# A delta-rule attention with two feed-forward networks: sums of squares in two reduced-precision parts, and the last output tile finished, copied and stored in parts

## The reference

```python
def _moe2_ref(x, w_gate, w_val, w_out, rms_g):        # x: 3072 x 384
    rms = np.sqrt(np.mean(x * x, axis=-1, keepdims=True) + 1e-06)
    xn = x / rms * rms_g
    g = xn @ w_gate                                   # 384 x 1536
    silu = g * (1.0 / (1.0 + np.exp(-g)))
    val = xn @ w_val                                  # 384 x 1536
    return (silu * val @ w_out).astype(np.float32)    # 1536 x 384
```

## Time and profile before

| | us |
|---|---|
| median of 3 executions | 1063.65 |
| the three executions | 1062.71, 1063.65, 1069.65 |
| the profiled execution, device time | 1068.47 |
| its span, first to last instruction | 1066.6 |
| TensorE busy in it | 1039.2 (97%) |
| VectorE busy | 535.0 (50%) |
| ACT busy | 468.8 (44%) |

### The profile page before, as it was taken

The page is one execution under the profiler, slowest core; times in us unless marked ns, Lnnn a source line. Parts: engine busy times, 40 slices in busy tenths (PEclk is TensorE's granted clock), DMA queues, the critical chain, the costliest instruction groups (busy, mean ns, idle before and its releaser), DMA issues.

```text
span 1066.6 us, 25024 instructions
## 1 busy us (share of the span) xinstructions
PE 1039.2 (97%) x11132; PEld 856.3 (80%) x11132; DVE 535.0 (50%) x1001; ACT 468.8 (44%) x843; POOL 9.6 (1%) x20
## 2 busy tenths in 40 slices
PE   8889899999999999999999999999999999999996
PEld 4469888777777877777778888888888888888885
DVE  6648667747846837753356444324333333333322
ACT  5744654574473474464466542232232232232211
POOL 1000000000000000000000000000000000000000
PEclk9889999999999999999999999999999999999999
DMA  9405102301500410030021230200200100100101
GB/s 258 133 2 130 22 3 62 89 3 37 115 2 3 120 31 3 32 119 3 28 93 49 70 119 1 60 1 1 60 1 13 48 1 1 30 1 1 30 1 30
DMA packets 19034, 48.09 MB, mean 45 GB/s; under 512 B 2448, under 2 KB 9232, under 8 KB 17872
## 3 DMA queue, kind: packets, MB, share of 16 engines
q1 hardware_dynamic: 18800, 46.11, 16.0%
q10 hardware_dynamic: 128, 0.39, 0.1%
HBM read 37.06 MB, written 9.44 MB: 44 GB/s over the span
## 4 chain that ended last, share of the span: by engine, by line
PE 92%; ACT 3%; DMA 2%; issue 1%; DVE 1%; SPq 0%; DVEq 0%; ACTq 0%
PE bank L713 21%; PE hps L1257 19%; PE acc L1272 19%; PE acc L732 10%; PE hps L713 7%; PE hps L732 4%; DMA stage<-w_in 1%; PE acc L1294 1%; PE bank L1216 1%; PE bank L1151 1%; PE bank L1180 1%; PE bank L1202 1%; PE bank L1195 1%; PE bank L1229 1%; PE bank L1141 1%
## 5 line engine op out<-in xcount | busy, mean ns | idle before, releaser
L630 ACT ACTIVATE g<-bank 128x512 f32<-128x512 f32 x72 | 43.2, 600 | 257.2 <-PE bank L713 142.6
L1257 PE MATMUL hps<-xh,w1h 128*128 128x512 f32 (+1 forms) x336 | 129.5, 385 | 2.7 <-DVE g L1089 2.1
L1272 PE MATMUL acc<-g1h,w2h 128*128 128x512 f32 (+1 forms) x336 | 127.0, 378 | 0.4 <-ACT x2s L941 0.3
L1257 PE MATMUL hps<-xl,w1h 128*128 128x512 f32 (+1 forms) x336 | 122.4, 364 | 0.0
L1257 PE MATMUL hps<-xh,w1l 128*128 128x512 f32 (+1 forms) x336 | 122.2, 364 | 0.0
L1272 PE MATMUL acc<-g1l,w2h 128*128 128x512 f32 (+1 forms) x336 | 122.0, 363 | 0.0
L1272 PE MATMUL acc<-g1h,w2l 128*128 128x512 f32 (+1 forms) x336 | 121.8, 363 | 0.0
L933 ACT ACTIVATE g1h<-g 128x512 fp32r<-128x512 f32 (+1 forms) x112 | 64.0, 571 | 120.6 <-DVE g L1089 105.5
L1097 DVE TENSOR_TENSOR g1l<-g,g1h 128x512 fp32r<-128x512 f32 (+1 forms) x112 | 68.6, 612 | 91.5 <-ACT g1h L933 91.1
L1089 DVE SCALAR_TENSOR_TENSOR g<-hps,g 128x512 f32<-128x512 f32 (+1 forms) x112 | 68.2, 609 | 61.6 <-ACT g L927 61.4
L924 ACT ACTIVATE g<-hps,half_c 128x512 f32<-128x512 f32 (+1 forms) x112 | 69.8, 623 | 54.0 <-PE hps L1257 53.2
(11 more groups left out here) (183 smaller groups left out, 2039.9 us busy)
## 6 DMA issues: line engine op xcount, KB each, us to landing
kqT<-kq SPq DMA_DIRECT2D x22, 384.0 KB, 6.6
v_in<-v SPq DMA_DIRECT2D x6, 768.0 KB, 4.3
k_in<-k SPq DMA_DIRECT2D x6, 768.0 KB, 5.6
x2d<-x2s SPq DMA_DIRECT2D x18, 256.0 KB, 5.2
x2t<-x2d SPq DMA_DIRECT2D x6, 768.0 KB, 5.5
y<-y_t SPq DMA_DIRECT2D x48, 96.0 KB, 2.2
stage<-w_in SPq DMA_DIRECT2D x4, 768.0 KB, 9.9
stage<-w_out SPq DMA_DIRECT2D x4, 768.0 KB, 7.6
```

The source lines that it names most:

```text
L630: act.activation(silu[:, f % 2, :], gps[f % 2][:, :], ACT.Silu).then_inc(e_silu, 1)
L1257: last = pe.matmul(hps[f % 2][:, 0:WIDTH[n]], wt[:, kk, P * f:P * f + P], xx[:, kk, COLS[n]], start=(kk == 0 and e == 0), stop=(kk == KD - ...
L1272: last = pe.matmul(acc[j][:, 0:WIDTH[n]], wt[:, f, P * j:P * j + P], gg[:, f % 2, 0:WIDTH[n]], start=(f == 0 and e == 0), stop=(f == NF1 - ...
```

## The change

The sum of squares goes through the high and low parts too. After `fold`, ACT copies the folded squares into an fp32r tile `sumh` (`sumhi`), VectorE subtracts it into `suml` (`sumlo`), and `sums` is two fp32r matmuls with fp32r ones in place of one fp32 matmul. The tile of ones is written by ACT at the start and no longer by POOL. In the last step, y of the last block runs the eight matmuls with `prh` first, behind a wait for `prh` alone, then the four with `prl`, each of which completes a group and signals it. VectorE copies groups 0 and 2, ACT groups 1 and 3; SP issues the four stores of the half m = 0, ACT those of m = 1.

```diff
@@ -260,8 +260,8 @@
     n = TILES - 1
     high, low = [("w2h", n, p) for p in range(15)], [("w2l", n, p) for p in range(15)]
     beside = {("h", n, 0): [("square", 0, 0)], ("h", n, 1): [("square", 0, 1)],
-              ("gl", n, 1): [("square", 0, 2), ("fold", 0, 0)],
-              ("h", n, 2): high[0:1], ("gl", n, 2): high[1:2] + low[0:2], ("h", n, 3): high[2:3], ("gl", n, 3): high[3:4] + low[2:4],
+              ("gl", n, 1): [("square", 0, 2), ("fold", 0, 0), ("sumhi", 0, 0)],
+              ("h", n, 2): high[0:1], ("gl", n, 2): high[1:2] + [("sumlo", 0, 0)] + low[0:2], ("h", n, 3): high[2:3], ("gl", n, 3): high[3:4] + low[2:4],
               ("o", n, 2): [("sums", 0, 0)], ("gl", n, 4): [("root", 0, 0)], ("h", n, 5): high[4:5],
               ("gl", n, 5): [("invert", 0, 0)], ("gl", n, 6): [("invert", 0, 1)], ("h", n, 7): high[5:6],
               ("gl", n, 7): [("scale", 0, 0)], ("h", n, 8): high[6:7], ("gl", n, 8): [("hi", 0, 0)] + low[4:6],
@@ -279,7 +279,7 @@
 def second_network():
-    norms = {2: ["square"], 3: ["fold"], 4: ["sums", "root"], 6: ["invert"], 7: ["invert"], 8: ["scale"], 9: ["hi"], 10: ["lo"]}
+    norms = {2: ["square"], 3: ["fold", "sumhi", "sumlo"], 4: ["sums", "root"], 6: ["invert"], 7: ["invert"], 8: ["scale"], 9: ["hi"], 10: ["lo"]}
     parts = {0: (15, 17), 1: (17, 19), 2: (19, 20), 3: (20, 21), 4: (21, 22), 5: (22, 24), 6: (24, 26), 7: (26, 27)}
     out = []
     for n in range(NSTEP):
@@ -322,7 +322,7 @@
         w2h = sb("w2h", [P, NF1, DM], F32R)
         w2l = sb("w2l", [P, NF1, DM], F32R)
         half_c = sb("half_c", [P, 1])
-        ones = sb("ones", [P, P])
+        ones = sb("ones", [P, P], F32R)
         eps_c = sb("eps_c", [P, 1])
         gain = sb("gain", [P, KD])
         x2s = sb("x2s", [P, KD, T])
@@ -375,9 +375,10 @@
         y_t = sb("y_t", [P, NT4, DM])
         xn0h = sb("xn0h", [P, KD, T], F32R)
         xn0l = sb("xn0l", [P, KD, T], F32R)
+        sumh, suml = sb("x2_sum_hi", [P, T], F32R), sb("x2_sum_lo", [P, T], F32R)
         e_gain, e_x, e_w = sem("gain_loaded"), sem_pair("x2_loaded"), sem_pair("w2_loaded")
         e_wh, e_wl = sem("w2_hi_ready"), sem("w2_lo_ready")
-        e_half, e_fold = sem("x2_half_folded"), sem("x2_folded")
+        e_half, e_fold, e_fh, e_fl = sem("x2_half_folded"), sem("x2_folded"), sem("x2_sum_high"), sem("x2_sum_low")
         e_sq, e_ss, e_rms, e_rinv, e_xs = (sem("x2_squared"), sem("x2_summed"), sem("rms_ready"), sem("rms_inverted"),
                                            sem("x2_normed"))
         w2_raw = {"gate": w_gate.rearrange("(k p) f -> p k f", p=P), "value": w_val.rearrange("(k p) f -> p k f", p=P),
@@ -463,7 +464,7 @@
             by_vector = {("GK", 0, 0): (s_gk2, 1), ("GK", 0, 1): (s_gk2, 2), ("U", 0, 0): (s_upd2, 1), ("PU", 0, 0): (s_y2, 1)}
-            N_CONST = 1 + MEM + 5
+            N_CONST = 1 + MEM + 4
             N_ZERO = 3
             N_NRM = 5
             N_INV = 2 + 2 * INV
@@ -553,6 +554,7 @@
             e_gv, e_silu, e_pr, e_prh, e_prl = (sem("gate_val_done"), sem("silu_ready"), sem("product_ready"),
                                                 sem("product_hi"), sem("product_lo"))
             e_y, e_yc, e_out = sem("y_done"), sem("y_copied"), sem("y_stored")
+            e_ylast, e_ya = sem("y_last_done"), sem("y_last_copied")
             y_rows = y_out.rearrange("(bp m s) n -> bp m s n", bp=BP, m=MEM)
             N_OUT = NT4 * MEM * 16
@@ -566,18 +568,32 @@
                     sp.wait_ge(e_xl, n - 1)
                 sp.dma_start(x2t[n % 2][:, :, :], x2d[n, :, :, :]).then_inc(e_x[n % 2], 16)
+
+            def y_store(eng, n, j, m):
+                hf, bp = j // BP, j % BP
+                eng.dma_start(y_rows[bp ^ m, m, n * STEP + hf * C:n * STEP + hf * C + C, :], y_t[C * m:C * m + C, j, :])\
+                    .then_inc(e_out, 16)
+
+            def last_out_ready(eng, j):
+
+                if j % 2:
+                    eng.wait_ge(e_ya, j // 2 + 1)
+                else:
+                    eng.wait_ge(e_yc, (NSTEP - 1) * NT4 + j // 2 + 1)
             def second_sync(sp):
                 load_x2(sp, 2)
                 load_x2(sp, 3)
                 for n in range(NSTEP):
                     for j in range(NT4):
-                        hf, bp = j // BP, j % BP
+                        if n == NSTEP - 1:
+                            last_out_ready(sp, j)
+                            y_store(sp, n, j, 0)
+                            continue
                         sp.wait_ge(e_yc, n * NT4 + j + 1)
                         for m in range(MEM):
-                            sp.dma_start(y_rows[bp ^ m, m, n * STEP + hf * C:n * STEP + hf * C + C, :], y_t[C * m:C * m + C, j, :])\
-                                .then_inc(e_out, 16)
+                            y_store(sp, n, j, m)
                     if n + 4 < NSTEP:
                         load_x2(sp, n + 4)
@@ -611,6 +627,9 @@
                         act.wait_ge(e_ss, n)
                     act.activation(x2sq[:, :, :], x2t[n % 2][:, :, :], ACT.Square).then_inc(e_sq, 1)
+                elif kind == "sumhi":
+                    act.wait_ge(e_fold, n + 1)
+                    act.activation(sumh[:, :], x2sq[:, 0, :], ACT.Copy).then_inc(e_fh, 1)
                 elif kind == "root":
                     act.wait_ge(e_ss, n + 1)
                     act.activation(rms[:, :], sums_of(n)[:, :], ACT.Sqrt, bias=eps_c[:, 0:1], scale=1.0 / DM).then_inc(e_rms, 1)
@@ -622,6 +641,14 @@
                 elif kind == "hi":
                     act.wait_ge(e_xs, n + 1)
                     act.activation(xnh[n % 2][:, :, :], x2t[n % 2][:, :, :], ACT.Copy).then_inc(e_xh, 1)
+                elif kind == "out" and n == NSTEP - 1:
+                    act.wait_ge(e_out, n * N_OUT)
+                    for j in range(1, NT4, 2):
+                        act.wait_ge(e_ylast, j + 1)
+                        act.activation(y_t[:, j, :], yps[j][:, 0:DM], ACT.Copy).then_inc(e_ya, 1)
+                    for j in range(NT4):
+                        last_out_ready(act, j)
+                        y_store(act, n, j, 1)
                 elif kind == "silu":
                     act.wait_ge(e_gv, n * NF2 + f + 1)
                     if n == 0 and f < 2:
@@ -654,6 +681,9 @@
                     dve.tensor_tensor(x2sq[:, 0, :], x2sq[:, 0, :], x2sq[:, 1, :], ALU.add).then_inc(e_half, 1)
                     dve.wait_ge(e_half, n + 1)
                     dve.tensor_tensor(x2sq[:, 0, :], x2sq[:, 0, :], x2sq[:, 2, :], ALU.add).then_inc(e_fold, 1)
+                elif kind == "sumlo":
+                    dve.wait_ge(e_fh, n + 1)
+                    dve.tensor_tensor(suml[:, :], x2sq[:, 0, :], sumh[:, :].bitcast(F32), ALU.subtract).then_inc(e_fl, 1)
                 elif kind == "invert":
                     invert_rms(dve, n, f)
                 elif kind == "scale":
@@ -673,6 +703,11 @@
                     dve.wait_ge(e_prh, n * NF2 + f + 1)
                     dve.tensor_tensor(prl[:, f % 2, :], pr[:, f % 2, :], prh[:, f % 2, :].bitcast(F32), ALU.subtract).then_inc(e_prl, 1)
+                elif kind == "out" and n == NSTEP - 1:
+                    dve.wait_ge(e_out, n * N_OUT)
+                    for j in range(0, NT4, 2):
+                        dve.wait_ge(e_ylast, j + 1)
+                        dve.tensor_copy(y_t[:, j, :], yps[j][:, 0:DM]).then_inc(e_yc, 1)
                 elif kind == "out":
                     dve.wait_ge(e_y, (n + 1) * NF2)
                     if n:
@@ -684,11 +719,12 @@
             def second_tensor(pe, u):
                 kind, n, f = u
                 if kind == "sums":
-                    pe.wait_ge(e_fold, n + 1)
+                    pe.wait_ge(e_fl, n + 1)
                     if n:
                         pe.wait_ge(e_pr, (n - 1) * NF2 + 4)
-                    pe.matmul(sums_of(n)[:, :], ones[:, :], x2sq[:, 0, :], start=True, stop=True).then_inc(e_ss, 1)
+                    pe.matmul(sums_of(n)[:, :], ones[:, :], sumh[:, :], start=True, stop=False)
+                    pe.matmul(sums_of(n)[:, :], ones[:, :], suml[:, :], start=False, stop=True).then_inc(e_ss, 1)
                 elif kind == "gv":
                     if f == 0:
                         pe.wait_ge(e_xl, n + 1)
@@ -725,6 +761,15 @@
                         pe.wait_ge(s_g, NF1 * TILES)
                         pe.wait_ge(s_x2, KD * TILES)
+                    if (n, f) == (NSTEP - 1, NF2 - 1):
+                        pe.wait_ge(e_prh, NSTEP * NF2)
+                        for j in range(NT4):
+                            for wt in (woh, wol):
+                                pe.matmul(yps[j][:, 0:DM], prh[:, f % 2, P * j:P * j + P], wt[:, f, :], start=False, stop=False)
+                        pe.wait_ge(e_prl, NSTEP * NF2)
+                        for j in range(NT4):
```

(4 more changed lines are left out.)

## The result

| 20 executions each | before | changed |
|---|---|---|
| median, us | 1064.3 | 1059.18 |
| lowest and highest, us | 1062.71, 1069.95 | 1056.96, 1066.54 |
| profiled execution: device time, span | 1068.47, 1066.6 | 1058.23, 1056.4 |

The ratio of the executions is 0.9946, with an interval of 0.9931 to 0.9961: the changed kernel is 4.2 to 7.3 us faster. That is measurable, and under 1%. The forecast was 1059.0. One execution of the kernel before, taken beside e1 to e4, lasted 5689.6 us in a slow state, and the ratios of those runs leave it out.

What follows compares the result with a forecast made beforehand. TensorE, busy 97% of the span, was taken to bound the kernel, apart from the 7.6 us end. Sums 2.0 plus end 2.7 gave 4.7 us off the 1063.65 median: 1059.0 us, range 1057.2 to 1064.6.

Steps and rivals of the forecast that it cites:

- The sums: On TensorE, two fp32r matmuls replace each two-pass fp32 matmul: 0.40 us saved each, counted in five of six, 2.0 us.
- Rivals 2 and 3: Sums: 2, root holds TensorE in steps 1 to 4, 1060.6 us, chance 0.08; 3, matmuls no cheaper, 1061.0 us, 0.05.
- The new operations at nothing: sumhi (0.63 us) on ACT and sumlo (0.69) on VectorE fit in idle time in the steps and last round, costing nothing.
- The end: After the last matmuls: an earlier first group and stores issued by SP and ACT together save 2.7 us.
- The earlier group: Last y: high-part matmuls start before the low part is ready, so group 0 is ready 1.2 us earlier.
- near 1: Sign at the end: with ACT's four stores beside SP's, the DMA share would be near 1.
- At full use without a gap, from 1059.5, that is 1063.1: Last stores: sixteen DMA engines need 3.6 us from 1059.5; with thin start, landing and close the span ends at 1063.95.
- by issue alone: Last stores: four issues each on SP and ACT, ACT's last at 1060.9, landing at 1063.1; span ends at 1063.5.
- the sign of being wrong that the prediction named: Last stores: the forecast is wrong if the landing grows beyond 2.5 us as the stores crowd.
- Rival 1: Last stores stay serial, each issue taking twice as long when two run; end gains only 1.2, 1060.5 us, chance 0.15.
- The forecast's own range: Whole kernel: 1057.3 to 1060.3 us, from an end gain of 1.2 to 3.7 and a shorter execution 0.9 below the median.
- Rival 4: Lowered clock in the first 80 us: if two of three timed executions are long, about 1064.4 us, chance 0.2.

Runs made afterwards that it cites:

- e1: The sums in two parts alone, with the end as in the kernel before; median 1063.54 us of 10, ratio to the kernel before 0.9982.
- e4: Changed kernel, but the last y and VectorE's four copies as before; SP and ACT issue four stores each; 1059.21 us, one execution, end 11.08 us.
- e5: Changed kernel, but the last step's eight stores carry 192 of 384 columns, half the bytes; 1059.15 us, one execution, end 9.55 us.
- e3: Changed kernel, but SP issues all eight stores of the last step, ACT none; 1060.22 us, one execution, end 11.98 us.
- e11: Changed kernel with last chain in halves, step 0 weight piece moved, VectorE copying all groups, groups 0 and 2 each one 128-partition store; 1065.44 us of 12.
- e9: Changed kernel with the last block's chain in halves of 256 tokens and a step 0 weight piece moved from f = 4 to 5; 1058.31 us of 6.

## Why the prediction was right

**The sums.** 0.39 for each, five of six kept, and the sixth lost to root in step 0: forecast 5 x 0.40 = 2.0, measured 0.4 + 1.63 = 2.0. Rivals 2 and 3 did not come: 0.46 of room is left in step 1 (0.42 forecast), and an fp32r matmul with ones starts 0.23 ahead of the next like any other.

**The new operations at nothing.** Right in both places; the last round has 1.4 us to spare (1.3 forecast). The e1 trace shows the sums' change alone cost nothing elsewhere.

**The end.** Right in its mechanism, 0.5 too small: 3.16 for 2.7. The earlier group gave 1.1 to 1.2, as forecast, and the share of the engines was 0.97 ("near 1"). The term that was mis-sized is the one I chose between two: "At full use without a gap, from 1059.5, that is 1063.1", which took the 3.6 us of the engines' work as a fixed amount. With two queues the same stores took 2.7. The other term, by issue alone, gave an end 10.05 after the start of the last gate/value matmul (1063.5 - 1053.45); it was 9.99. It came out so by two errors against each other, which is luck. I had ACT issue only after its copies, at 5.55; it began at 4.99, beside its running copy, and its last issue stood 0.35 earlier than I had it. The landing took 2.5, not 2.2, and 2.6 at most: the sign of being wrong that the prediction named, a landing over 2.5, was just reached. With half the bytes it was 2.0 (e5) and with one issuer 2.2 (e3), so the crowding that it feared was there, at a cost of 0.3.
Rival 1 (serial stores) is refuted by e3 and e4: two issuers at once each keep some 0.6 an issue. The sentence of the Trainium skill that the prediction cites ("DMA: Bandwidth & Descriptors", Issuing engines are not separate DMA queues), that a second issuer saves the sequencer's time only, holds for the source of most of the gain and not for its size: it calls that time usually small, and here it was 2.0 us. The traces show in addition that the engines moved 283 to 294 GB/s with two queues and 145 to 155 with one (e3).

**The sum and the clock.** 5.2 by the traces, 5.1 by the medians, 4.7 forecast. That the measured 1059.18 lies so near the forecast 1059.0 is luck in part: the gain was 0.4 to 0.5 larger than forecast, and the kernel before took 1064.3 as the median of 20 executions, 0.65 more than the 1063.65 of three from which the forecast started. The two cancel. The forecast's own range is also added up a little too narrow: by the terms it names it runs from 1057.0 (1063.65 - 2.0 - 3.7 - 0.9) to 1060.5, and not from 1057.3 to 1060.3; the measured time lies in both. Rival 4 was real as a spread: executions of either kernel reach 1066 to 1070 us, and in the changed kernel's they are those with the lower mean clock. It decided no median: of 20 executions 3 of the changed kernel are above 1063. That the long executions are a group 5.9 above the others was much to read from four. Of the 20, four do stand apart (1069.26 to 1069.95), but beside the experiments executions of the same kernel lie in between (1067.03, 1067.62, 1068.60).

## What to carry to other kernels

At a kernel's end count the issues as well as the bytes: eight stores in a row from one engine lasted 5 us where the data took 2.7 with two issuers, and splitting them over two engines brought more (2.0) than finishing the first group earlier (1.2). Where single executions differ by more than the change, cut both traces at the same instructions; stretches that the clock doesn't touch repeat within 0.15 us. And when an engine has both to copy and to issue, put nothing that waits ahead of its issues.

## What the runs showed of the hardware

- A store of 64 partitions x 1536 bytes took 0.6 us to issue on SP and on ACT (median of four each; 0.47 to 0.8 singly), with half its bytes 0.59 and 0.61, and of 128 partitions 0.57 (e11, two of them). So an issue's price went neither by bytes nor by partitions.
- Stores through two queues kept the sixteen engines busy for 2.7 us, through one for 3.6, at the same 0.79 MB. Why the work gets less was not settled.
- ACT issued a transfer while its own copy was still running (issue at 1051.40, copy until 1051.85 in the changed kernel), but in e9 not ahead of a wait that stands before it in its program (1052.47).
- A store whose target's slowest dimension is 2 ran on two of the sixteen engines, at 49 GB/s, and held up the issues behind it for up to 2.9 us.
- An fp32 matmul of 128x512 cost TensorE 0.86 us at the full clock, two fp32r matmuls in its place 0.47.
